# Attention and two mixing layers on one core: the first batch's Fourier transform moves into the attention loop

## The chip, the cores and the metric

One core of a Trainium2 chip runs the whole program. The metric is the device time in microseconds (us) of one execution. TensorE is PE in the profile's rows (its weight loads are PEld), VectorE is DVE, ScalarE is ACT, GpSimd is POOL, and SyncE, which here only issues DMAs, is SP. Each engine works through its own instructions strictly in order, and they meet at semaphores.

## The reference

Three layers follow one another. The first is attention over two batches of eight heads, in which a query sees only the keys that fall into the same bucket of a hash:

```python
q_bits = (np.einsum('bhsd,dk->bhsk', q, proj) > 0)          # 6 bits; the same for k
mask = q_bucket[:, :, :, None] == k_bucket[:, :, None, :]
scores = np.where(mask, scale * q @ k^T, -1e9)              # S = 768, D = 64
attn = softmax(scores);  x = attn @ v                       # x: (2, 768, 512)
X = np.real(np.fft.fft(np.fft.fft(x, axis=1), axis=2))      # second layer
u = x + X;  un = (u - mean) / sqrt(var + 1e-6)              # by row
x = u + np.maximum(un @ w_ch1, 0) @ w_ch2                   # 512 -> 2048 -> 512
theta = x @ w_theta; zr = x * cos(theta); zi = x * sin(theta)   # third layer
u = x + w_tok_r @ zr + w_tok_i @ zi;  out = u + np.maximum(u @ w_ch, 0)
```

## The kernel before

All products are made of three fp32r matmuls: each operand is split into a high part and a low part, and `product` adds high times high, high times low and low times high. So nearly every tile is evicted from PSUM twice: ACT writes the high part, then DVE subtracts it from PSUM to get the low one.

**The attention loop.** `schedule()` writes one list of slots that PE, ACT, DVE and POOL all walk. There is a slot for each of the 96 tiles (16 heads of 6 tiles of 128 queries) and six more to drain; below, (h, t) is tile t of head h, and (16, t) are the draining slots. In a slot PE computes the scores of its tile (four matmuls, lines 771 and 772), transposes the exponentials of the tile two slots earlier (`eta` and `etb`, three transposes each, line 746), does a third of the product with v (lines 786, 787), and then the small units of that slot: `bits` (the hash products, in (h, 0) and (h, 1) for the next head) and `back` (transposing the result, in (h, 3) and (h, 5) for the head before). DVE takes the row maximum straight from the score bank (`negmax`, line 993), makes the tiny `affine` out of it (line 996) and evicts the low halves `ETL`; ACT takes the exponential `E` (line 626) and evicts the high halves `ETH`. `eta`, `etb`, `bits` and `back` go round a ring of three PSUM banks (4, 5, 6).

**Between the heads.** POOL scales q (line 492), splits q and k into `TOPH` and `TOPL` two heads ahead (lines 500, 502, slot t = 2), turns the evicted products `MB` into the mask rows `MR` (line 507, slot t = 1), adds up the result and writes it into `X` (`finish`, lines 516 and 519), and splits v. SP moves the pieces with DMAs from one buffer to another: `move_away`, the load of the next q and k, `move_in`, `move_mask` (`QM<-MR`, `KM<-MR`, lines 426 and 427), the load of v. A head's scores wait for its mask rows.

**Tables and W1.** In slots t = 2 and t = 5 POOL issues one DMA out of the list `early`: twelve tables of sines and cosines, then the four DMAs of 1 MB that fill `W1H`.

**The transform.** After the loop both batches are transformed one after the other. By batch: DVE folds `X` (`fold_add`, `fold_even`, `fold_odd`), ACT and DVE split it into `EH`, `EL`, `OH`, `OL`; stage one is five groups of matmuls into `TH` and `TL` (`TG = 5`); stage two is three times a cosine and a sine product, of whose difference and sum (`DS`) DVE updates `X`. The second batch is folded while the first is in stage one.

**Into the second layer's matmuls.** SP stages W1 and W2 in chunks of 256 KB (two buffers), from which POOL makes the low halves: `split_low(n_w1)` for the sixteen chunks of W1, then `rstd` of six rows of tiles (lines 573, 575), then `load_high("w2")` (four DMAs of 1 MB, line 486) and `split_low` for W2. PE starts the second layer only with

```python
            pe.wait_ge(s_high["w1"], 16 * len(highs["w1"]))
            pe.wait_ge(s_low, n_w1)
            for n in range(2, CH):
                norm_transpose(n)
```

and the first `shrink` (the product with W2) waits for the first chunk of `W2L`.

## Time and profile before

| | |
|---|---|
| runs | 804.74 us median of 3 (799.62 to 807.62) |
| profiled execution | 805.94 us, span 803.8 us |
| PE busy | 745.3 us, 93% of the span |
| DVE, ACT, POOL busy | 445.5, 318.3, 286.9 us |
| attention loop | from the first scores at 14.11 us to 262 us |
| transform | 262 us to 330.75 us, where the first matmul with W1 starts |
| second layer | 330.75 us to about 600 us, third layer to the end |

The busy time of PE is read with care: the ends of pipelined matmuls are modelled, so that neighbours overlap in the rows. Whether PE waits is seen by the idle time in brackets behind a row, and what a matmul costs by the distance to the next one. Everything after 331 us depends only on when it starts.

### The profile page before, as it was taken

What the parts mean: (1) busy time and instruction counts of PE and PEld (TensorE: products, weight loads), DVE (VectorE), ACT (ScalarE), POOL (GpSimd) and SP (SyncE); (2) the same over time, 40 slices, a digit from 0 to 9 for tenths busy, and PEclk for the clock granted to TensorE, in tenths of its full rate; (3) what the DMA queues carried; (4) which work ended last, traced back from release to release, by engine and by line L of the source; (5) the groups of instructions that cost most, each with busy time, mean ns of one, the idle gap of its engine ahead of it and who ended that gap; (6) DMA issues with size and microseconds to landing.
All of it is one profiled execution on the core that took longest, in us unless ns stands there. A gap on an engine that the chain in (4) does not pass through costs nothing.

```text
span 803.8 us, 10972 instructions
## 1 busy us (share of the span) xinstructions
PE 745.3 (93%) x3826; PEld 625.6 (78%) x3826; DVE 445.5 (55%) x770; ACT 318.3 (40%) x659; POOL 286.9 (36%) x275
## 2 busy tenths in 40 slices
PE   4999989989999769799999999999995998999998
PEld 2788888878898557688888888888874787888876
DVE  2998997889998688522212122211127565855433
ACT  2889887879899211211111111011014342322201
POOL 3788977668772376335000000200002114312100
PEclk9999999999999869799999999999998999999999
DMA  5366548733430134712000001300002231000002
GB/s 146 94 154 170 136 93 203 192 89 87 113 73 5 53 114 135 210 40 78 1 1 1 0 1 47 99 0 1 1 31 81 60 92 40 1 14 21 19 27 78
DMA packets 44679, 56.25 MB, mean 70 GB/s; under 512 B 15956, under 2 KB 27860, under 8 KB 44116
## 3 DMA queue, kind: packets, MB, share of 16 engines
q1 hardware_dynamic: 38100, 41.65, 19.3%
q0 software_dynamic: 6528, 13.92, 6.1%
q8 instruction: 32, 0.52, 0.3%
q14 instruction: 19, 0.16, 0.1%
HBM read 38.65 MB, written 3.15 MB: 52 GB/s over the span
## 4 chain that ended last, share of the span: by engine, by line
PE 75%; DVE 14%; issue 4%; DMA 3%; ACT 2%; POOL 1%; SPq 1%; ACTq 0%; POOLq 0%
PE PS L724 20%; PE PS L726 19%; PE PS L725 19%; DVE negmax L993 4%; PE PS L746 3%; DVE ETL L1003 3%; PE PS L786 3%; PE PS L771 2%; PE PS L772 2%; PE PS L787 2%; DVE affine L996 2%; DMA KM<-MR 2%; PE PS L907 1%; PE PS L914 1%; PE PS L757 1%
## 5 line engine op out<-in xcount | busy, mean ns | idle before, releaser
L1113 DVE SCALAR_TENSOR_TENSOR HL<-PS,HH 128x512 fp32r<-128x512 f32 x48 | 33.2, 692 | 188.6 <-ACT HH L687 188.6
L687 ACT ACTIVATE HH<-PS 128x512 fp32r<-128x512 f32 x48 | 28.7, 598 | 210.4 <-PE PS L726 210.4
L626 ACT ACTIVATE E<-PS,affine 128x768 f32<-128x768 f32 x96 | 95.3, 992 | 35.7 <-DVE affine L996 33.0
L993 DVE TENSOR_REDUCE negmax<-PS 128x1 f32<-128x768 f32 x96 | 90.9, 947 | 28.4 <-PE PS L772 27.5
L1003 DVE TENSOR_TENSOR ETL<-PS,ETH 128x384 fp32r<-128x384 f32 x192 | 97.1, 545 | 1.2 <-ACT ETH L619 1.2
L619 ACT ACTIVATE ETH<-PS 128x384 fp32r<-128x384 f32 x192 | 83.4, 488 | 9.6 <-PE PS L746 9.0
L746 PE MATMUL PS<-ident,E 128*128 128x128 f32 x576 | 82.1, 276 | 4.2 <-DVE ETL L1003 4.2
L771 PE MATMUL PS<-TOPH,TOPL 128*128 128x512 f32 x192 | 69.8, 364 | 9.4 <-DMA KM<-MR 9.1
L724 PE MATMUL PS<-UTH,W1H 128*128 128x512 f32 x192 | 76.8, 400 | 1.7 <-DVE UTL L1096 1.7
L786 PE MATMUL PS<-ETH,VHL 128*128 128x384 f32 x192 | 73.2, 381 | 4.9 <-ACT OS L635 4.0
L725 PE MATMUL PS<-UTL,W1H 128*128 128x512 f32 x192 | 75.9, 396 | 0.0
L726 PE MATMUL PS<-UTH,W1L 128*128 128x512 f32 x192 | 75.8, 395 | 0.0
L726 PE MATMUL PS<-W2H,HL 128*128 128x512 f32 x192 | 74.7, 389 | 0.0
L724 PE MATMUL PS<-W2H,HH 128*128 128x512 f32 x192 | 74.7, 389 | 0.0
L725 PE MATMUL PS<-W2L,HH 128*128 128x512 f32 x192 | 74.7, 389 | 0.0
L746 PEld LDWEIGHTS PS<-ident,E 128*128 128x128 f32 x576 | 65.9, 141 | 7.6 <-DVE ETL L1003 7.1
L587 POOL TENSOR_TENSOR ZF<-X,SC 128x512 f32<-128x512 f32 x24 | 30.5, 1291 | 107.2 <-ACT SC L708 107.2
L787 PE MATMUL PS<-ETL,VHL 128*128 128x384 f32 x192 | 65.2, 340 | 0.0
L772 PE MATMUL PS<-KM,QM 76*128 76x512 f32 x192 | 63.3, 349 | 0.0
L724 PE MATMUL PS<-ZH,WTH 128*128 128x512 f32 x144 | 59.9, 416 | 0.0
L507 POOL TENSOR_SCALAR MR<-MB,gamma 24x768 fp32r<-24x768 f32 x15 | 44.0, 2933 | 43.6 <-ACT MB L643 43.6
L726 PE MATMUL PS<-ZH,WTL 128*128 128x512 f32 x144 | 57.0, 396 | 0.0
(167 smaller groups left out, 1530.2 us busy)
## 6 DMA issues: line engine op xcount, KB each, us to landing
stage<-in_moe_w_ch_dram SPq DMA_DIRECT2D x36, 256.0 KB, 2.6
QK<-in_qk_dram SPq DMA_DIRECT2D x16, 384.0 KB, 4.0
W1H<-in_moe_w_ch_dram POOLq DMA_DIRECT2D x4, 1024.0 KB, 10.4
W2H<-in_moe_w_ch_dram POOLq DMA_DIRECT2D x4, 1024.0 KB, 8.8
QM<-TOPH SPq DMA_DIRECT2D x16, 192.0 KB, 3.0
KM<-TOPL SPq DMA_DIRECT2D x16, 192.0 KB, 3.6
VR<-in_v_dram SPq DMA_DIRECT2D x16, 192.0 KB, 2.8
TOPL<-QM SPq DMA_DIRECT2D x16, 192.0 KB, 2.7
```

The lines of the kernel that those rows point to most:

```text
L619: nc.scalar.activation(ETH[:, t // HALF, k * HALF:(k + 1) * HALF, (t % HALF) * P:(t % HALF + 1) * P], bank, ACT.Copy).then_inc(s_eth, 1)
L626: nc.scalar.activation(E[:, tile % NE, :], s_bank(tile)[:, 0:S], ACT.Exp, bias=affine[:, t, 1:2], scale=affine[:, t, 0:1], accum_out=esum[ ...
L724: nc.tensor.matmul(dst, hl, hr, start=start, stop=False)
L725: nc.tensor.matmul(dst, hl, lr, start=False, stop=False)
L726: return nc.tensor.matmul(dst, ll, hr, start=False, stop=stop)
L746: last = nc.tensor.transpose(bank[:, j * P:(j + 1) * P], E[:, tile % NE, (first + j) * P:(first + j + 1) * P], ident[:])
L771: nc.tensor.matmul(dst, TOPL[:, h % 3, c], TOPH[:, h % 3, lo:hi], start=True, stop=False)
L772: last = nc.tensor.matmul(dst, QM[:, h % 2, c], KM[:, h % 2, lo:hi], start=False, stop=True)
L786: nc.tensor.matmul(OT, VHL[:, h % 2, j, :], ETH[:, c, j, :], start=(j == 0), stop=False)
L787: last = nc.tensor.matmul(OT, VHL[:, h % 2, j, :], ETL[:, c, j, :], start=False, stop=(j == QT - 1))
L993: nc.vector.tensor_reduce(negmax[:, t, 1:2], s_bank(tile)[:, 0:S], AX_X, ALU.max, negate=True).then_inc(s_max, 1)
L1003: nc.vector.tensor_tensor(ETL[where], blocks(ring(unit_no[kind, h, t])[:, 0:HC]), ETH[where].bitcast(F32), ALU.subtract).then_inc(emptied[ ...
```

## The change

Batch 0 of the transform leaves the stretch behind the loop and becomes units of the loop while batch 1's heads are computed. Its fold additions are DVE work of (9, 1), (9, 2) and (9, 4); the rest of the fold and the low halves are POOL work in (9, 5), (10, 0) and (10, 2); its stage one is `s1` units in (10, 4), (11, 1), (11, 2), (11, 4), (12, 1), its stage two an `edge` unit in (12, 4) and `sin` and `cos` units in heads 13 and 14. POOL updates `X` in (13, 3), (14, 2), (15, 0). The work buffers of batch 0 lie in the place of `W1H`, so the four DMAs of `W1H` are issued in (15, 1). The ring of three banks becomes fixed banks: `eta` 4, `etb` 5, every other unit 6. The two `bits` units of a head become one that puts both halves into one bank of 56 partitions, evicted once. SP loads q and k of head h + 2 after the mask rows of head h, where it loaded those of h + 1 before them; the mask rows take four DMAs of half the length. Behind the loop POOL makes the six `rstd` before it splits W1, and loads W2H after it, as before.

```diff
 def schedule():
-    slots = [(None, None, None, [("bits", 0, i) for i in range(2)])]
+    transform = {(10, 4): ("s1", 0, 0), (11, 1): ("s1", 0, 1), (11, 2): ("s1", 0, 2), (11, 4): ("s1", 0, 3), (12, 1): ("s1", 0, 4),
+                 (12, 4): ("edge", 0, 0)}
+    for i, place in enumerate(((13, 1), (13, 2), (13, 4), (14, 1), (14, 2), (14, 4))):
+        transform[place] = ("cos" if i % 2 else "sin", 0, i // 2)
+    slots = [(None, None, None, [("bits", 0, 0)])]
...
-        if h + 1 < NH and t < 2:
-            units.append(("bits", h + 1, t))
+        if h + 1 < NH and t == 0:
+            units.append(("bits", h + 1, 0))
...
+        if (h, t) in transform:
+            units.append(transform[h, t])
...
-        def ring(u):
-
-            return PS[:, 4 + u % RING, :]
-
-
+        bank_of = {"eta": 4, "etb": 5}
         OT = PS[:, 7, 0:HC]
+
+        def bank(kind):
+            return PS[:, bank_of.get(kind, 6), :]
...
             def move_in(h):
-                sp.wait_ge(s_ring, done["bits", h, 1])
+                sp.wait_ge(s_ring, done["bits", h, 0])
...
                 move_away(h)
-                if h + 1 < NH:
-                    load_qk(h + 1)
                 move_in(h)
                 move_mask(h)
+                if h + 2 < NH:
+                    load_qk(h + 2)
...
             def mask_rows(h):
-                pool.wait_ge(emptied["bits"], 2 * (h + 1))
-                pool.wait_ge(s_mask, 32 * h)
+                pool.wait_ge(emptied["bits"], h + 1)
+                pool.wait_ge(s_mask, 64 * h)
...
+            def fold_even(b):
+                pool.wait_ge(s_fold, 2 * HALF * (b + 1))
+                nc.gpsimd.tensor_tensor(FE[b][:, :, 1:LH], AE[b][:, :, 1:LH], AE[b][:, :, DM - 1:LH:-1], ALU.add).then_inc(s_even, 1)
+                nc.gpsimd.tensor_copy(FE[b][:, :, 0:LH + 1:LH], AE[b][:, :, 0:LH + 1:LH]).then_inc(s_even, 1)
...
+            def fold_low(b):
+                pool.wait_ge(s_eh, 3 * b + 2)
+                nc.gpsimd.tensor_tensor(EL[b][:, :, 0:LH + 1], FE[b][:, :, 0:LH + 1], EH[b][:, :, 0:LH + 1].bitcast(F32),
+                                        ALU.subtract).then_inc(s_el, 1)
...
+            def update(b, t):
...
+                pool.wait_ge(s_ds, 2 * n + 2)
+                nc.gpsimd.tensor_tensor(lower, lower, DS[b][:, n % 2, :, 0:LH + 1], ALU.add).then_inc(s_u, 1)
+                nc.gpsimd.tensor_tensor(upper, upper, DS[b][:, n % 2, ::-1, 1:LH], ALU.add).then_inc(s_u, 1)
...
-            early = [(dst, src, s_table) for dst, src in tables] + [(dst, src, s_high["w1"]) for dst, src in highs["w1"]]
+            early = [(dst, src, s_table) for dst, src in tables]
...
+                if (h, t) == (9, 5):
+                    fold_even(0)
+                if (h, t) == (10, 0):
+                    fold_odd(0)
+                if (h, t) == (10, 2):
+                    fold_low(0)
+                if (h, t) in ((13, 3), (14, 2), (15, 0)):
+                    update(0, ((13, 3), (14, 2), (15, 0)).index((h, t)))
+                if (h, t) == (15, 1):
+                    pool.wait_ge(s_ring, done["cos", 0, HALF - 1])
+                    pool.wait_ge(s_u, 2 * HALF)
+                    load_high("w1")
             finish(NH - 1, 1)
+            for n in range(QT):
+                row_scale(n)
             pool.wait_ge(s_pv, 2 * NH)
             split_low(n_w1)
...
+            pool.wait_ge(s_t, TG)
+            load_high("w2")
+            pool.wait_ge(s_m, 4)
+            pool.wait_ge(s_fix, 2 * B)
+            split_low(n_w2, FT // 2)
...
-            def take_bank(u):
-
-                if u >= RING:
-                    old = units[u - RING]
-                    pe.wait_ge(emptied[old[0]], nth[old])
...
+                if previous[name] is not None:
+                    pe.wait_ge(*freed(previous[name]))
...
+                    r = h % 3
+                    product(on[0:MP, 0:HC], projH[:, 0:MP], TOPH[:, r, 0:HC], projL[:, 0:MP], TOPL[:, r, 0:HC], True, False)
+                    last = product(on[0:MP, 0:HC], projH[:, 32:PROJ], TOPH[:, r, HC:S], projL[:, 32:PROJ], TOPL[:, r, HC:S], False, True)
...
+                elif kind == "s1":
+                    m = WIDTHS[i]
+                    pe.wait_ge(s_table, 16 * len(tables))
+                    pe.wait_ge(s_eh, 3)
+                    pe.wait_ge(s_el, 3)
+                    last = (even_group if i < HALF else odd_group)(on[0:m, 0:KC], 0, i)
...
+                place = divmod(slot - 1, QT)
+                if place in ((9, 1), (9, 2), (9, 4)):
+                    fold_add(0, ((9, 1), (9, 2), (9, 4)).index(place))
+                if place == (9, 4):
+                    fold_edge(0)
...
+                if place == (15, 1):
+                    dve.wait_ge(s_ns, 1)
+                    fix_edge(0, FX)
+                if (15, 2) <= place < (16, 2):
+                    row_moments(slot - 1 - 15 * QT - 2)
```

On POOL, between two splits of v, at the turn from head 9 to head 10. Before:

```order
L537 TENSOR_TENSOR VHL<-VR,VHL 128x6x64
L516 TENSOR_TENSOR OS_68<-OL_67 128x192
L519 TENSOR_TENSOR X<-OS_68,einv 128x3x64
L507 TENSOR_SCALAR MR<-MB,gamma 24x768
L492 TENSOR_SCALAR QK<-QK 64x768
L500 CAST TOPH<-QK 128x768
L502 TENSOR_TENSOR TOPL<-QK,TOPH 128x768
```

And in the changed kernel, behind the same split of v:

```order
L547 TENSOR_TENSOR FE_114<-AE_112 128x3x255
L548 COPY FE_114<-AE_112 128x3x2
L583 TENSOR_TENSOR OS_68<-OL_67 128x192
L586 TENSOR_TENSOR X<-OS_68,einv 128x3x64
L551 TENSOR_TENSOR FO_115<-AO_113 128x3x255
L543 TENSOR_SCALAR MR<-MB,gamma 56x384
L528 TENSOR_SCALAR QK<-QK 64x768
L536 CAST TOPH<-QK 128x768
L538 TENSOR_TENSOR TOPL<-QK,TOPH 128x768
L555 TENSOR_TENSOR EL_117<-FE_114,EH_116 128x3x257
L557 TENSOR_TENSOR XL<-FX,XH 1x257
L559 TENSOR_TENSOR OL_119<-FO_115,OH_118 128x3x255
```

Two operations of the fold stand around `finish`, and the three low halves behind the split of q and k.

On PE, slot (10, 4) of the changed kernel, from its transposes on, followed by the scores of (10, 5):

```order
L847 MATMUL PS<-ident,E 128x128 x6
L902 MATMUL PS<-ETH,VHL 128x384
L903 MATMUL PS<-ETL,VHL 128x384
...
L811 MATMUL PS<-ALT,XH 128x386
L812 MATMUL PS<-ALT,XL 128x386
L805 MATMUL PS<-CSH,EH_116 128x386
L806 MATMUL PS<-CSL,EH_116 128x386
L807 MATMUL PS<-CSH,EL_117 128x386
...
L887 MATMUL PS<-TOPH,TOPL 128x512
```

The first group of stage one now stands in PE's row ahead of the next tile's scores; before, the scores follow directly upon line 787.

On POOL, from the last `finish` to W2. Before:

```order
L519 TENSOR_TENSOR X<-OS_68,einv 128x3x64
L528 TENSOR_TENSOR W1L<-stage,W1H 128x512 x16
L573 TENSOR_SCALAR rstd<-moments 128x1
L575 TENSOR_TENSOR rstd<-rstd,mhalf 128x1
...
L486 DMA W2H<-in_moe_w_ch_dram 128x4x512 x4
L528 TENSOR_TENSOR W2L<-stage,W2H 128x512 x8
```

In the changed kernel:

```order
L586 TENSOR_TENSOR X<-OS_68,einv 128x3x64
L572 TENSOR_SCALAR rstd<-moments 128x1
L574 TENSOR_TENSOR rstd<-rstd,mhalf 128x1
...
L595 TENSOR_TENSOR W1L<-stage,W1H 128x512 x16
L522 DMA W2H<-in_moe_w_ch_dram 128x4x512 x4
L595 TENSOR_TENSOR W2L<-stage,W2H 128x512 x8
```

The six pairs of `rstd` have moved from behind the sixteen splits to the front of them.

## Rows read from the trace of the kernel before

**Rows 1.** Windows: start:end, length, busy us (instructions) by engine, granted clock, DMA share, GB/s.
```profile
220.00:240.00 20.00, 19.77 (x134) 18.08 (x133) 18.57 (x35) 18.27 (x43) 13.88 (x11) 1.00 0.31 76
262.00:331.00 69.00, 50.44 (x239) 39.09 (x239) 54.09 (x86) 14.94 (x31) 36.98 (x37) 0.80 0.41 130
```

**Rows 2.** Timeline of PE: scores of (12, 5) and of (13, 0).
```profile
213.34 0.40 PE L771 MATMUL PS<-TOPH,TOPL 128*128 128x512 f32 x1
...
216.12 0.48 PE L771 MATMUL PS<-TOPH,TOPL 128*128 128x512 f32 x1
```

**Rows 3.** Timeline of POOL: the mask rows made in heads 6, 10 and 11.
```profile
111.15 2.93 POOL L507 TENSOR_SCALAR MR<-MB,gamma 24x768 fp32r<-24x768 f32 x1 [4.32 <-ACT MB L643]
...
179.00 2.93 POOL L507 TENSOR_SCALAR MR<-MB,gamma 24x768 fp32r<-24x768 f32 x1 [5.20 <-ACT MB L643]
...
193.61 2.93 POOL L507 TENSOR_SCALAR MR<-MB,gamma 24x768 fp32r<-24x768 f32 x1 [2.91 <-ACT MB L643]
```

**Rows 4.** Timeline of POOL and the chain of waits, heads 7 to 9.
```profile
118.97 0.62 POOL L561 DMA_DIRECT2D W1H<-in_moe_w_ch_dram  x1
...
150.64 2.13 POOL L492 TENSOR_SCALAR QK<-QK 64x768 f32<-64x768 f32 x1 [3.78 <-DMA QK<-in_qk_dram]
...
130.74 4.54 DMA KM<-MR
```

**Rows 5.** Timelines of POOL and DVE: the split of k beside `affine`.
```profile
99.94 1.82 POOL L502 TENSOR_TENSOR TOPL<-QK,TOPH 128x768 fp32r<-128x768 f32 x1
...
100.08 1.69 DVE L996 SCALAR_TENSOR_TENSOR affine<-negmax 128x2 f32<-128x2 f32 x1
...
215.29 0.80 DVE L996 SCALAR_TENSOR_TENSOR affine<-negmax 128x2 f32<-128x2 f32 x1
```

**Rows 6.** Timeline of SP: issue of the first mask rows.
```profile
10.84 0.83 SPq L426 DMA_DIRECT2D QM<-MR  x1
```

**Rows 7.** Timeline of PE: batch 1's stage one and stage two, first and last matmul.
```profile
303.82 0.44 PE L815 MATMUL PS<-ALT,XH 1*128 1x386 f32 x1
...
313.52 0.34 PE L726 MATMUL PS<-SSH,OL 128*127 128x386 f32 x1
...
316.15 0.37 PE L724 MATMUL PS<-CDH,TH 128*128 128x258 f32 x1
...
323.54 0.28 PE L726 MATMUL PS<-SDH,TL 127*128 127x258 f32 x1
```

**Rows 8.** Timeline of DVE: batch 0's fold, first and last but one.
```profile
262.66 1.75 DVE L952 TENSOR_TENSOR AE<-X 128x1536 f32<-128x1536 f32 x1
...
269.54 0.41 DVE L972 TENSOR_TENSOR XL<-FX,XH 1x257 fp32r<-1x257 f32 x1
```

**Rows 9.** Groups of instructions, whole span: POOL's high parts, DVE's `row_moments`.
```profile
L500 POOL CAST TOPH<-QK 128x768 fp32r<-128x768 f32 x15 | 12.3, 823 | 1.0
...
L1030 DVE BATCH_NORM_STATS2 stats<-X 128x6 f32<-128x512 f32 x12 | 8.1, 677 | 0.0
```

**Rows 10.** Timeline of PE: a start after a wait, and the last product with v.
```profile
135.52 0.76 PE L771 MATMUL PS<-TOPH,TOPL 128*128 128x512 f32 x1 [1.59 <-DMA KM<-MR]
...
265.33 0.34 PE L787 MATMUL PS<-ETL,VHL 128*128 128x384 f32 x1
```

**Rows 11.** Timeline of POOL behind the loop.
```profile
276.25 2.53 POOL L528 TENSOR_TENSOR W1L<-stage,W1H 128x512 fp32r<-128x512 f32 x2 [2.75 <-DMA stage<-in_moe_w_ch_dram]
...
309.94 0.23 POOL L573 TENSOR_SCALAR rstd<-moments 128x1 f32<-128x1 f32 x1
...
315.68 3.10 POOL L486 DMA_DIRECT2D W2H<-in_moe_w_ch_dram  x4
329.89 2.68 POOL L528 TENSOR_TENSOR W2L<-stage,W2H 128x512 fp32r<-128x512 f32 x2 [11.11 <-issue]
```

**Rows 12.** Timeline of PE: the first matmuls with W1 and with W2.
```profile
330.75 0.76 PE L724 MATMUL PS<-UTH,W1H 128*128 128x512 f32 x1 [1.70 <-DVE UTL L1096]
...
339.19 0.39 PE L724 MATMUL PS<-W2H,HH 128*128 128x512 f32 x1
```

More of the change, by code:

```diff
@@ L128, in program @@
     TOPL = put("TOPL", [P, 3, S], F32R)
+    MX = put("MX", [1, 2, DM])
+    assert used[0] <= dft_at + 4 * 4 * QT * KC
     used[0] = dft_at + 4 * 4 * QT * KC
@@ L220, in program @@
             units += us
-        unit_no = {u: i for i, u in enumerate(units)}
-        done = {}
+        done, previous, last_on = {}, {}, {}
         for u in units:
             done[u] = len(done) + 1
+            k = bank_of.get(u[0], 6)
+            previous[u] = last_on.get(k)
+            last_on[k] = u
         nth, seen = {}, {}
@@ L251, in program, with freed @@
         s_x = sem("s_x")
+        def freed(u):
+            if u[0] in emptied:
+                return emptied[u[0]], nth[u]
+            return {"s1": (s_tl, nth[u]), "sin": (s_bs, nth[u]), "cos": (s_ds, 2 * nth[u]), "edge": (s_ns, 1)}[u[0]]
         s_mr = sem("s_mr")
@@ L439, in _ @@
             load_v(1)
+            load_qk(2)
             n = 0
@@ L642, in _ @@
                             act.wait_ge(s_mr, h - 1)
[L643 removed]
+                        nc.scalar.activation(MB[:], bank(kind)[0:MP, 0:HC], ACT.Copy).then_inc(emptied["bits"], 1)
                     elif kind == "back":
@@ new lines, in _ @@
+                if slot - 1 == 10 * QT + 1:
+                    high_even(0)
+                if slot - 1 == 10 * QT + 2:
+                    high_odd(0)
+            high_even(1)
+            high_odd(1)
+            for g in range(TG):
+                m = WIDTHS[g]
+                act.wait_ge(s_t, g + 1)
+                nc.scalar.activation(TH[1][0:m, g, :], PS[0:m, g % 2, 0:KC], ACT.Copy).then_inc(s_th, 1)
+            for t in range(HALF):
+                n = HALF + t
+                act.wait_ge(s_m, t + 1 + (t > 0))
+                act.wait_ge(s_ds, 2 * (n - 1))
+                nc.scalar.activation(BS[1][:, n % 2, 0:LH + 1], PS[:, 4 + n % 2, 0:LH + 1], ACT.Copy).then_inc(s_bs, 1)
@@ new lines, in _ @@
+            for g in range(TG):
+                m = WIDTHS[g]
+                pe.wait_ge(s_eh, 3 + (2 if g < HALF else 3))
+                pe.wait_ge(s_el, 3 + (2 if g < HALF else 3))
+                if g >= 2:
+                    pe.wait_ge(s_tl, TG + g - 1)
+                (even_group if g < HALF else odd_group)(PS[0:m, g % 2, 0:KC], 1, g).then_inc(s_t, 1)
+            pe.wait_ge(s_th, TG * B)
+            pe.wait_ge(s_tl, TG * B)
+            pe.wait_ge(emptied["back"], seen["back"])
+            pe.wait_ge(emptied["pv"], 2 * NH)
@@ new lines, in _ @@
+            for g in range(TG):
+                m = WIDTHS[g]
+                dve.wait_ge(s_th, TG + g + 1)
+                nc.vector.tensor_tensor(TL[1][0:m, g, :], PS[0:m, g % 2, 0:KC], TH[1][0:m, g, :].bitcast(F32), ALU.subtract).then_inc(s_tl, 1)
+                if g < 2:
+                    normalize(g)
+            normalize(2)
+            normalize(3)
+            for t in range(HALF):
+                n = HALF + t
+                two = X[:, QT + t:2 * QT:HALF, :]
+                lower, upper = two[:, :, 0:LH + 1], two[:, :, DM - 1:LH:-1]
+                differences(1, t, PS[:, 2 + n % 2, :])
+                dve.wait_ge(s_ds, 2 * n + 2)
+                nc.vector.tensor_tensor(lower, lower, DS[1][:, n % 2, :, 0:LH + 1], ALU.add).then_inc(s_u, 1)
+                nc.vector.tensor_tensor(upper, upper, DS[1][:, n % 2, ::-1, 1:LH], ALU.add).then_inc(s_u, 1)
+                if t == 0:
+                    dve.wait_ge(s_m, 2)
+                    fix_edge(1, PS[0:1, 1, :])
```

410 lines of the change are left out of this document (193 added, 217 removed).

## The prediction

> **What bounds the kernel now.** I read the windows first. In a head of the loop that nothing disturbs, PE is busy 19.77 of 20 us, DVE 18.57, ACT 18.27 and POOL 13.88, at the full clock of 2.4 GHz [rows 1]: the loop is bound by PE, and DVE stands close behind (about 1.0 us free in a head). Then the timeline of POOL's mask rows, as a metronome: one head lasts 14.61 us (179.00 to 193.61), but the four before it took 67.85 us (111.15 to 179.00) where 58.44 were due: 9.4 us of waiting [rows 3]. The chain of waits and POOL's timeline name the cause: the first DMA of W1H is issued at 118.97, then mask rows take 4.54 us to land and a load of q and k holds POOL for 3.78 us [rows 4]. Last, the stretch behind the loop, 262 to 331 us: PE is busy 50.44 of 69 us at a mean granted clock of 0.80, POOL 36.98 [rows 1]. The reader is to see there which engine would be last if the first batch's transform were gone: not PE, as worked out below.
>
> **Part 1, what enters the loop.** PE: stage one of a batch took 303.82 to 313.7, 9.9 us, and stage two 316.15 to 323.7, 7.5 us, both at the full clock [rows 7]. PE has next to no idle time in the loop, so these 17.4 us are paid in full. The evictions of these units on ACT and DVE (stage one 0.5 us each, estimated from the widths) stand in slots that the units themselves lengthen by 1 to 2.3 us; I put them at 0. POOL's six updates of X, some 1.2 us each by TOPL's 1.82 us for 768 columns [rows 5], lie in POOL's free time: 0 as well, between 0 and 4 us.
>
> Head 9: DVE gets the additions, 2 times 1.75 us in all [rows 8], and some 0.8 us for the edge row: 4.3 us in a head with 1.0 us free, so 3.3 us on the path. Bounds 1 (the tiles in flight absorb part) and 6 (each addition also waits for POOL, next part but one).
>
> Slot (10, 4): PE's first stage-one group waits for `OL`, the last of a row of POOL work that starts when DVE has done its additions of (9, 4), about when head 10 begins. In POOL's order: FE 1.9, `finish` 1.1, FO 1.8, MR 1.5 (half of 2.93, as half the columns), QK 2.13, TOPH 0.82, TOPL 1.82, EL 1.85, XL 0.6, OL 1.8; the fold's operations priced by TOPL's rate, `finish` as two of 192 columns [rows 3, 4, 5, 9]. That is 15.3 us. PE reaches its place after 11.8 us: head 12 began at 216.12 less 14.61 = 201.51, and its sixth tile's scores stand at 213.34 [rows 2]. PE waits 3.5 us, and everybody behind it: the scores of (10, 5) are queued after that group. Bounds 1 and 7. After a wait of 1.59 us the first matmul took 0.76 us instead of 0.40 [rows 2, 10], the low clock of 1.2 GHz; I add 1.7 us for that, between 0 and 5.
>
> Head 15: `row_moments` of four tiles at 0.68 us [rows 9] and the repair of the edge row give DVE 3.5 us, while PE there has no hash products: 1.5 us, between 0 and 3.5.
>
> The start: before the first scores the mask rows need two more DMA issues at 0.83 us [rows 6]: 1.6 us. Later heads don't pay it, as the rows come earlier: one `bits` unit instead of two, and 1.5 us of MR instead of 2.93 [rows 3]. The single eviction of MB saves ACT, which is not the bound: 0.
>
> **Part 2, what leaves the loop.** The four DMAs of W1H, and with them the 9.4 us of waiting [rows 3, 4]. The loads of q and k move behind the mask rows of SP's row, so the mask rows pass one transfer of 384 KB earlier and q and k arrive a head before their use. The tables stay where they are. At 100.08 an `affine` of two columns took 1.69 us, until POOL's split at 99.94 had ended [rows 5]; that split now falls elsewhere in the head, and I count half of those 1.5 us as gone. Together 10.2 us saved; bounds 7 and 12.5.
>
> Loop: 17.4 + 3.3 + 3.5 + 1.7 + 1.5 + 1.6 - 10.2 = +18.8 us.
>
> **Part 3, behind the loop** (in the old trace's times, as if the loop ended at the same time). The last product with v ends at 265.7 [rows 10]. ACT is no longer blocked by the first batch's fold, so two evictions, a transpose and `finish` complete X at about 268.5 (2.8 us, an estimate). Then two rows run side by side.
>
> PE's: the fold of batch 1, which batch 0's stage one no longer hides, 262.66 to 269.95 before, 7.3 us [rows 8], gives 275.8; from the first stage-one matmul to the first with W1 it was 303.82 to 330.75, 26.9 us [rows 7, 12]; with 2 us for a low clock at the start, 304.7.
>
> POOL's: six `rstd`, 309.94 to 315.68, 5.7 us, to 274.2; sixteen splits of W1, 276.25 to 309.94, 33.7 us, to 307.9 [rows 11]. This is later than PE's row, and PE may transpose its last two tiles only behind it: some 3.6 us more, 311.5, and the two first `hidden` groups take 330.75 to 339.19, 8.4 us [rows 12]: ready for W2 at 319.9. But POOL issues W2H only behind those splits: it took 315.68 to 329.89, 14.2 us, to land, and the first split 1.3 us [rows 11]. So the first matmul with W2 stands at 323.4 instead of 339.19 [rows 12]: 15.8 us saved, less 1.7 us for a low clock after a 3.5 us wait: -14.1 us. Of the 28 us and more that a batch's transform costs behind the loop, the other half goes to POOL's row, which is as long as before and only starts earlier.
>
> **Sum.** 18.8 - 14.1 = +4.7 us. The profiled execution took 805.94 us (span 803.8 and 2.1 around it) and would take 810.6. It lies 1.2 us above the median, so the prediction for the median is 804.74 + 4.7 = 809.4 us.
>
> **A rule that speaks against the change.** What the row shows: an `affine`, which reads two small tiles in SBUF, took 1.69 us beside POOL's TOPL and ended with it, and 0.80 us in the undisturbed head [rows 5]. The change puts eleven more such operations on POOL, and six additions with two SBUF inputs on DVE, into the loop; I priced what they may hold up by the bounds of head 9 and by rival A. The Trainium skill ("SBUF — State Buffer", section "Who interferes with whom") says that a VectorE instruction with two SBUF inputs and a GpSimd instruction that reads SBUF exclude each other, the later one blocking until the other has ended; the row at 100.08 agrees. If it holds for every one of the eleven, the result is rival A's.
>
> **The rivals.**
> A, slower: `affine` is held up more often. `eta` and `etb` used to have a third bank to run into; now the transposes of a tile wait for DVE's eviction of the tile before, so that a delay on DVE reaches PE one unit sooner. For it: DVE is free only 1.0 us in a head, TOPL lasts 1.82 us of a slot that has 14.61 / 6 = 2.4, and it meets other tiles than before, since MR starts a slot earlier and is 1.5 us shorter [rows 1, 3, 5]. Against it: POOL has 1.5 us less in each head. From about 0.6 us a head it decides; at that, 14 heads lose 8.4 us: 818 us.
> B, faster by the loop: fold and low halves fit in, 1 us in head 9 and 1 us at (10, 4) with no low clock, none in head 15, and 12.5 us of waits go. Loop +8.5, behind it -15.8 as PE keeps its clock: 797.5 us.
> C, POOL's row is not last: without competition for SBUF from DVE the sixteen splits go at 1.26 us each and the loads keep up, ending by 300. Then PE's row decides, W1 at 304.7, W2H lands by 314.5: first W2 matmul at 316, 7 us earlier: 802 us. Against it: the splits wait for the staging DMAs (2.75 us before the first [rows 11]), not for POOL alone.
> D, the units don't run beside anything: nothing else is gained at all, W1's waits return with the table DMAs. That is +9.4 on the forecast, 819 us; little speaks for it.
>
> **How the numbers follow.** Forecast 0.47, A 0.22, B 0.17, C 0.10, D 0.04. The forecast's own range is 803 to 815. A measurement of this kernel tells a change of about 1%, 8 us, from none: under 796.7 is faster, over 812.8 slower. B falls half on either side of 796.7 and widens it downwards: faster 0.13. A and D and the upper end of the forecast are slower: 0.33. Same 0.54. The range takes in most of A and B: 797 to 819.
>
> **What would show it.** The mask rows' metronome is even from head 2 on, without the gaps of 111 to 179 us. In slot (10, 4) PE waits for POOL's `OL` by 3 to 4 us, and not before. Head 9 lasts about 18 us. Between the loop and W1's first matmul PE waits for POOL's last split of W1, with an idle time of 5 us or more, and the first matmul with W2 waits for `W2L`. The first matmul with W1 stands 49 to 50 us behind DVE's last eviction of the loop (68 before). I would be wrong if the heads' period moves by more than 0.5 us, or if the splits of W1 end before PE's row does.

## The result, and the profile after

The changed kernel takes 827.92 us (median of 4 runs, 824.28 to 829.34), the kernel before 805.59 us (median of 4) beside it. The ratio is 1.028, 95% interval 1.022 to 1.035: 2.8% slower, outside the range of the prediction. The profiled execution took 829.34 us, its span is 826.8 us against 803.8 and its mean granted clock 0.963 against 0.968.

Four marks cut both traces at the same places: the mask rows (`MR` on POOL) as the metronome of the heads, the last product with v, the first matmul with W2, the end. Times in us:

| stretch | before | after | difference | forecast |
|---|---|---|---|---|
| start to the mask rows of (1, 1) | 35.02 | 38.57 | +3.55 | +1.6 |
| heads 1 to 8 | 125.24 | 124.26 | -0.98 | -6.1 |
| heads 9 to 13 | 77.17 | 98.87 | +21.70 | with the next row |
| (14, 1) to the last product with v | 27.90 | 36.88 | +8.98 | +23.3, both rows |
| to the first matmul with W2 | 73.86 | 61.56 | -12.30 | -15.8 |
| to the end | 464.6 | 466.7 | +2.1 | +1.7 |

(The forecast of -10.2 for the waits is divided by where the waits lay: 5.3 us of the 9.4 in heads 6 to 8 and the `affine` in head 5, the other 4.1 in head 9.) The loop lost 33.25 us where 18.8 were forecast; the stretches behind it gained 10.2 where 14.1 were forecast. Most of the 2.1 us at the end is the low clock behind PE's wait for W2: 0.60 from 360 to 364 us, where it was 1.00 before. Heads 1 to 8 show the loss best, since they have nothing of the transform in them. Timeline of POOL in the changed kernel, the mask rows made in slots (4, 1), (5, 1), (9, 1) and (10, 1):

```profile
85.20 1.65 POOL L543 TENSOR_SCALAR MR<-MB,gamma 56x384 fp32r<-56x384 f32 x1 [1.79 <-ACT MB L712]
100.73 1.65 POOL L543 TENSOR_SCALAR MR<-MB,gamma 56x384 fp32r<-56x384 f32 x1 [1.78 <-ACT MB L712]
...
162.83 1.66 POOL L543 TENSOR_SCALAR MR<-MB,gamma 56x384 fp32r<-56x384 f32 x1 [1.79 <-ACT MB L712]
186.15 1.66 POOL L543 TENSOR_SCALAR MR<-MB,gamma 56x384 fp32r<-56x384 f32 x1 [1.37 <-ACT MB L712]
```

A head lasts 15.53 us (85.20 to 100.73), and heads 1 to 8 all lie between 15.50 and 15.56; before it was 14.61 [rows 3]. So the gaps are gone, as forecast, and 0.92 us more in every head have taken their place. (One more gap is gone, of 2.6 us in head 5, which the prediction did not count: before, the mask rows of (5, 1) and (6, 1) stand at 93.91 and 111.15, ahead of the first DMA of W1H.) Head 9, with the fold additions, lasts 23.32 us.

Inside such a head, timeline of PE: the first matmul of the scores of (4, 1), behind the bits unit, to that of (5, 1), and one wait between them:

```profile
84.41 0.39 PE L887 MATMUL PS<-TOPH,TOPL 128*128 128x512 f32 x1
...
86.47 0.39 PE L887 MATMUL PS<-TOPH,TOPL 128*128 128x512 f32 x1
...
88.87 0.39 PE L887 MATMUL PS<-TOPH,TOPL 128*128 128x512 f32 x1
...
91.17 0.48 PE L887 MATMUL PS<-TOPH,TOPL 128*128 128x512 f32 x1
...
92.34 1.01 PE L847 MATMUL PS<-ident,E 128*128 128x128 f32 x6 [0.23 <-DVE ETL L1101]
...
93.90 0.39 PE L887 MATMUL PS<-TOPH,TOPL 128*128 128x512 f32 x1
...
96.74 0.48 PE L887 MATMUL PS<-TOPH,TOPL 128*128 128x512 f32 x1
...
99.93 0.39 PE L887 MATMUL PS<-TOPH,TOPL 128*128 128x512 f32 x1
```

The reader is to see the distances: 2.06, 2.40, 2.30, 2.73, 2.84, 3.19 us. A slot in which PE waits for nothing and that holds no unit is 2.06; a `back` adds 0.24, the six matmuls of the bits 1.04. Six slots, two `back` and the bits make 13.88 us, so PE stands still for 1.65 us of the head, against 0.73 before by the same count. DVE in the same head:

```profile
85.31 0.96 DVE L1091 TENSOR_REDUCE negmax<-PS 128x1 f32<-128x768 f32 x1 [0.95 <-PE PS L888]
...
89.77 0.96 DVE L1091 TENSOR_REDUCE negmax<-PS 128x1 f32<-128x768 f32 x1 [0.31 <-PE PS L888]
90.76 1.05 DVE L1094 SCALAR_TENSOR_TENSOR affine<-negmax 128x2 f32<-128x2 f32 x1
...
97.73 0.96 DVE L1091 TENSOR_REDUCE negmax<-PS 128x1 f32<-128x768 f32 x1 [0.67 <-PE PS L888]
```

DVE waits 0.95 us for scores, with all six bits matmuls in front of them on PE, and again 0.31 and 0.67; then PE waits for DVE. Neither has more work than before; they take turns in waiting. The table of waits, whole span, what waited, for whom, us, times, longest:

```profile
ACT E L698 <- DVE affine L1094: 43.3, 31, 14.8
DVE negmax L1091 <- PE PS L888: 40.0, 39, 8.3
...
PE PS L847 <- DVE ETL L1101: 12.6, 21, 3.3
...
PE PS L887 <- DMA KM<-MR: 7.3, 1, 7.3
```

PE's transposes wait for `ETL` 12.6 us in 21 places. For the mask rows PE waits once, before the first scores, and no longer in the middle as in [rows 10].

Head 9, timelines of DVE, POOL and PE:

```profile
175.34 1.51 DVE L1041 TENSOR_TENSOR AO<-X 128x512 f32<-128x512 f32 x1
176.77 0.40 DVE L1049 TENSOR_TENSOR FX<-X 1x255 f32<-1x255 f32 x1
177.11 1.76 DVE L1050 COPY FX<-X 1x2 f32<-1x2 f32 x1
...
176.93 1.92 POOL L547 TENSOR_TENSOR FE<-AE 128x765 f32<-128x765 f32 x1 [0.63 <-DVE AO L1041]
...
180.78 1.54 PE L847 MATMUL PS<-ident,E 128*128 128x128 f32 x6 [3.27 <-DVE ETL L1101]
```

A copy of two numbers on one partition took 1.76 us, until POOL's fold had ended, where the same copy takes 0.15 us behind the loop. After the wait of 3.27 us PE's matmuls run at the low clock of 1.2 GHz until 186.6 us (0.52 us for a bits matmul instead of 0.34).

Behind the loop, timelines of PE and POOL (with the last product with v, PE's wait for the last split of W1, the last `finish` and the third `rstd`):

```profile
298.58 0.33 PE L903 MATMUL PS<-ETL,VHL 128*128 128x384 f32 x1
...
309.94 0.66 PE L811 MATMUL PS<-ALT,XH 1*128 1x386 f32 x1 [9.83 <-DVE XL L1157]
...
344.72 1.94 PE L914 MATMUL PS<-ident,UN 128*128 128x128 f32 x8 [10.78 <-POOL W1L L595]
...
348.41 0.76 PE L805 MATMUL PS<-UTH,W1H 128*128 128x512 f32 x1 [1.74 <-DVE UTL L1185]
...
360.14 0.47 PE L805 MATMUL PS<-W2H,HH 128*128 128x512 f32 x1 [3.40 <-POOL W2L L595]
```

```profile
301.38 0.51 POOL L586 TENSOR_TENSOR X<-OS,einv 128x192 f32<-128x192 f32 x1
301.98 0.72 POOL L572 TENSOR_SCALAR rstd<-moments 128x1 f32<-128x1 f32 x1
...
305.53 2.70 POOL L572 TENSOR_SCALAR rstd<-moments 128x1 f32<-128x1 f32 x1
...
312.94 2.49 POOL L595 TENSOR_TENSOR W1L<-stage,W1H 128x512 fp32r<-128x512 f32 x2
...
344.30 3.12 POOL L522 DMA_DIRECT2D W2H<-in_moe_w_ch_dram  x4
358.74 2.50 POOL L595 TENSOR_TENSOR W2L<-stage,W2H 128x512 fp32r<-128x512 f32 x2 [11.33 <-DMA W2H<-in_moe_w_ch_dram]
```

These answer to [rows 7, 11, 12]. POOL's row is the last, step for step as forecast: PE waits 10.78 us for the last split of W1 and 3.40 us for `W2L`. Only the `rstd` took 11.0 us (301.98 to 312.94), not 5.7: the first four pairs, each one column wide, stand beside DVE's fold.

### The profile page after: what moved, and what is told of

It is laid out like the page before. It is cut to its first block, busy times and chain, and to the rows that moved or that the text cites. A ratio compares the mean times of both kernels' runs of the same rounds, so it can differ in the third digit from the quotient of the medians.

```text
span 826.8 us, 10977 instructions
## 1 busy us (share of the span) xinstructions
PE 752.6 (91%) x3826; PEld 628.8 (76%) x3826; DVE 431.7 (52%) x765; ACT 317.5 (38%) x645; POOL 284.2 (34%) x287
## 4 chain that ended last, share of the span: by engine, by line
PE 60%; POOL 20%; issue 11%; DMA 5%; DVE 2%; SPq 1%; ACT 1%; POOLq 0%
PE PS L805 18%; PE PS L807 17%; PE PS L806 17%; POOL QK L528 3%; DMA stage<-in_moe_w_ch_dram 3%; POOL TOPL L538 2%; POOL MR L543 2%; POOL OS L583 2%; PE PS L847 2%; POOL W1L L595 1%; DMA W2H<-in_moe_w_ch_dram 1%; POOL VHL L604 1%; POOL TOPH L536 1%; PE PS L998 1%; POOL X L586 1%
## 5 line engine op out<-in xcount | busy, mean ns | idle before, releaser
L847 PE MATMUL PS<-ident,E 128*128 128x128 f32 x576 | 87.3, 284 | 12.7 <-DVE ETL L1101 12.6
L847 PEld LDWEIGHTS PS<-ident,E 128*128 128x128 f32 x576 | 65.4, 144 | 23.3 <-DVE ETL L1101 22.3
L806 PE MATMUL PS<-ZL,WTH 128*128 128x512 f32 x144 | 56.8, 395 | 0.0
```

Of the source, the lines that this page charges most:

```text
L806: nc.tensor.matmul(dst, hl, lr, start=False, stop=False)
L847: last = nc.tensor.transpose(on[:, j * P:(j + 1) * P], E[:, tile % NE, (first + j) * P:(first + j + 1) * P], ident[:])
```

## The experiments

In the diffs lines of either kernel are cut to what changes. The head period is always the distance of the mask rows; "heads" are those without transform work.

### Which part makes the head longer

**Fixed banks alone, in the kernel before.**

```diff
-            return PS[:, 4 + u % RING, :]
+            return PS[:, bank_of.get(units[u][0], 6), :]
...
-                if u >= RING:
-                    old = units[u - RING]
+                old = previous[units[u]]
+                if old is not None:
```

> The kernel before with one part of the change alone: eta always in bank 4, etb in bank 5, bits and back in bank 6, in place of the ring of three. Theory 1 (the fixed banks cost the 0.92 us by which every undisturbed head grew, 15.53 against 14.61 us between two mask rows): the heads of this kernel grow by 0.6 to 1.0 us and the time by 10 to 15 us, to 816 to 821 us. Theory 2 (the heads grew because POOL's split of q and k now meets other affines, through the one bits unit and the shorter mask rows): nothing of that is in this kernel, the heads stay at 14.6 us and the time at 804 to 808 us.

808.96 us, ratio 1.005 (1.001 to 1.010). The period is 15.31 us, +0.70, in most heads and 15.4 to 15.6 in the others, as theory 1 had it, but the time is not: it gave 816 to 821 us. The gaps of 111 to 179 us vanish in the longer heads, so that the whole costs only 4 us; in the profiled execution, the fastest of this kernel, the last product with v even stands at 264.44, 0.9 us earlier than in [rows 10]. Fixed banks alone make a head longer, and a longer head hides late mask rows.

**The ring of three back, in the changed kernel** (`4 + k`, `k = len(done) % 3`, for all units; the bits stay one unit).

> The changed kernel with the ring of three banks given back to all units, the transform's too. Theory 1: heads 2 to 8 fall from 15.53 to 14.6 us, and the later ones by as much or more; 828 us become 811 to 816 us. Theory 2: 826 to 829 us, heads unchanged.

825.08 us, ratio 1.027 (1.019 to 1.036); heads 15.54 us as before the edit. So the banks are not all that holds the changed kernel's heads: something else gives the same period by itself.

**Both bits units in one slot, in the kernel before.**

```diff
-        if h + 1 < NH and t < 2:
-            units.append(("bits", h + 1, t))
+        if h + 1 < NH and t == 0:
+            units += [("bits", h + 1, 0), ("bits", h + 1, 1)]
```

> The kernel before, with one edit: both bits units of a head stand in slot t = 0 on PE, where the second stood in t = 1. Ring of three, two evictions, 24 mask rows and everything else stay. Theory 2a (the slots of PE are now uneven: a slot with six more matmuls of 384 columns lets ACT and DVE run dry and the next ones are short): heads go from 14.61 us towards 15.5 us, the time to 812 to 818 us. Theory 2b (not the place on PE but the merged bank, its 56 partitions and POOL's row behind it cost the 0.9 us a head): heads stay at 14.6 us, the time within 3 us of before.

819.87 us, ratio 1.025 (1.020 to 1.030); heads 16.0 to 16.3 us, more than either theory gave. The same matmuls and evictions, one slot earlier, cost 1.4 to 1.7 us a head. (Two units in one slot also go round the ring in another order, so part of it may be the ring's.)

**Ring of three and two bits units, in the changed kernel** (schedule, tiles of 24 rows, two evictions and two mask DMAs as in the kernel before).

> The changed kernel with the ring of three banks and with the two bits units of before (t = 0 and t = 1, 24 mask rows, two evictions, two mask DMAs); transform of the first batch in the loop, q and k two heads ahead, late W1H as in the changed kernel. Theory 2 (merging the bits, by place or by phase, costs the 0.9 us a head once the banks are a ring again): heads at 14.61 us, time 825 less 14 times 0.93, about 812 us. Rival (something else of the change, for instance q and k two heads ahead, moves POOL's row): heads stay at 15.5 us, time 825 us.

822.31 us, ratio 1.028 (1.022 to 1.033). Heads 14.6 to 14.9 us: with both undone the period is the old one, so that q and k loaded two heads ahead and late W1H have no part in its growth. (The four mask DMAs and the mask rows of 56 partitions were undone with the merged unit and were not tried alone.) But the ratio did not move, for heads 9 and 10 grew to 23.7 and 25.6. Timeline of PE in slot (10, 4) of this kernel:

```profile
188.59 0.65 PE L809 MATMUL PS<-ALT,XH 1*128 1x386 f32 x1 [6.05 <-POOL OL L557]
```

This is the wait that the prediction priced at 3.5 us, and the low clock behind it (0.65 us). In the changed kernel the same matmul waits 0.36 us: its own heads are late enough to hide it.

**POOL's split one slot later** (`scale_q` and `split_top` behind `finish` in t = 3; ring of three, one bits unit).

> The changed kernel with the ring of three banks and one unit of bits, and with POOL's scaling of q and its split of q and k one slot later (t = 3, behind finish). Theory 2b (phase: POOL's TOPL of 1.82 us meets an affine and holds it up at the point where PE has least in hand): heads change by 0.3 us or more in either direction, most likely back towards 14.6, time 812 to 820 us. Theory 2a (PE's uneven slots): heads stay at 15.5 us within 0.1, time 823 to 827 us.

823.67 us, ratio 1.029 (1.024 to 1.034); heads 15.53 to 15.77 but for one of 17.0 and one of 14.9. Which `affine` POOL's split holds up is not what sets the period; whether it would be shorter if none were held up was not tried.

**Two bits units, fixed banks kept, in the changed kernel.**

> The changed kernel with the fixed banks kept and only the bits unit undone: two units in t = 0 and t = 1 as before, both in bank 6. Theory (fixed banks are enough for a longer head: with two banks for eta and etb each transpose waits for DVE's eviction of the tile before): heads 15.3 us as with fixed banks in the kernel before, time 823 to 828 us. Rival (in the changed kernel the bits unit alone sets the head): heads at 14.6 to 14.9 us, time 814 to 820 us.

836.43 us, ratio 1.040 (1.033 to 1.046), slower than the changed kernel. Heads 15.3 to 15.5 us, as the theory had it for them; but PE waits 6.06 us for `OL` in (10, 4), and in five places, 5.4 us in all and 1.21 us at most, for the eviction of `MB`, since a bits unit now follows another unit in bank 6, and heads 9 to 13 take 110.3 us instead of 98.9. I had not thought of that bank.

Together: fixed banks give 15.3, the single bits unit 15.5, both 15.53, neither 14.61. Each is enough and they don't add.

### Heads 9 and 10

**Stage one a little later, in the changed kernel** (first group in (11, 1) instead of (10, 4), the others behind it).

> The changed kernel with the five stage-one units moved to (11,1), (11,2), (11,4), (12,1), (12,2), so that the first of them no longer follows POOL's low halves by less than a slot. If PE's place at (10,4) cost what was forecast (3.5 us and a low clock), 3 to 5 us are gained: 823 to 825 us. If the cost of heads 9 and 10 lies in DVE's additions and in what POOL holds up, POOL's low halves ending early enough for a PE that is late anyway, the time stays within 2 us of 828 us.

827.26 us, ratio 1.030 (1.023 to 1.037), and 99.0 us for heads 9 to 13 instead of 98.9: nothing. The forecast wait of 3.5 us in (10, 4), with its 1.7 us of low clock, is not where this kernel loses.

**The fold additions one to a slot, in the changed kernel.**

```diff
-                if place in ((9, 1), (9, 2), (9, 4)):
-                    fold_add(0, ((9, 1), (9, 2), (9, 4)).index(place))
-                if place == (9, 4):
+                if (9, 1) <= place < (10, 1):
+                    fold_add(0, *divmod(slot - 1 - 9 * QT - 1, 2))
+                if place == (10, 1):
                     fold_edge(0)
```

with POOL's fold in (10, 1), (10, 3), (10, 5) and stage one from (11, 1).

> The changed kernel (fixed banks, one bits unit, rstd behind the loop) with the six fold additions one to a slot in (9, 1) to (10, 0), the edge row in (10, 1), POOL's fold in (10, 1), (10, 3), (10, 5) and stage one from (11, 1). Theory P (head 9 is long because two additions in a row, and three ops on the edge row, stand between an affine and the next eviction, and PE has no bank to run into): heads 9 and 10 together take 35 to 38 us instead of 43.2, time 820 to 824 us. Rival (DVE's work is what it is, 4.3 us or more with the blocking, in a head that is full): heads 9 and 10 together 41 to 43 us, time as the changed kernel, 825 to 828 us.

823.69 us, ratio 1.028 (1.021 to 1.034). Heads 9 and 10 take 18.46 and 20.16, 38.6 us together instead of 43.2: between the two expectations. The two numbers are not quite alike, for this edit also moves a stage-one group out of (10, 4). Over heads 9 to 13, out of which nothing moves, it is 94.1 us instead of 98.9, and instead of 99.0 in the kernel with stage one later and nothing else: in the traces 4.8 us came from bunching. The measured times cannot confirm it, since the intervals of the two ratios overlap almost wholly.

### The DMAs

**W1H late, in the kernel before** (its four DMAs issued in (15, 1)).

> The kernel before with one part of the change alone: the four DMAs of W1H are issued in slot (15,1) instead of slots 2 and 5 of heads 7 and 8. If those DMAs caused the 9.4 us of waiting between 111 and 179 us of the trace before, the time falls by 7 to 10 us to 796 to 799 us and the mask rows come every 14.6 us from there on. Rival: the waiting stems from the loads of q and k, issued right ahead of the mask rows, and W1H only adds to it: less than 4 us are gained.

800.35 us, ratio 0.996 (0.991 to 1.000), above the 796 to 799 expected. The gaps of W1H are gone, one of 4.1 us stays between the mask rows of (5, 1) and (6, 1), where 2.6 us stood before. The last product with v stands 7.0 us earlier than in [rows 10] (258.31), the first matmul with W2 6.2 us earlier than in [rows 12] (333.00).

**W1H late and q and k two heads ahead, in the kernel before** (with a load for head 2 ahead of the loop).

```diff
                 move_away(h)
-                if h + 1 < NH:
-                    load_qk(h + 1)
                 move_in(h)
                 move_mask(h)
+                if h + 2 < NH:
+                    load_qk(h + 2)
```

> The kernel before with W1H loaded in (15, 1) and with q and k loaded two heads ahead behind the mask rows, nothing else. Theory (the gap of 4.1 us that late W1H alone left in head 6 is q and k coming late behind the table DMAs; loaded a head earlier they are there): all heads within 0.4 us of 14.6, the last mask rows at about 226 us, the time 4 us below late W1H alone: 794 to 799 us, ratio 0.988 to 0.994. Rival (the DMAs of the tables hold up whatever load or mask row stands beside them): a gap of 3 us or more stays in heads 4 to 7, ratio 0.994 to 0.999.

796.74 us (796.51 without one execution of 4127 us), ratio 0.994 (0.990 to 0.998, without that one), the lowest ratio here, though its interval overlaps almost wholly with that of W1H late alone. All heads from 2 on are 14.6 to 14.9 us, the last mask rows stand at 225.64 instead of 237.43: 11.8 us saved in the loop, where the forecast had 10.2. In the profiled execution (803.31 us, at the upper end of this kernel's) 5.0 us are left at the first matmul with W2 (334.23 against 339.19), where W1H late alone had left 6.2. What differs in between is the clock: 0.70 on average in the 69 us from 250.2, where [rows 1] have 0.80 for as long a stretch. The longest waits of PE there are nearly the same as before, among them 4.87 us for ACT's `OS` (4.88 before). What held the clock down was not tested.

### Behind the loop

**`rstd` in the loop, in the changed kernel** (`row_scale` in (15, 3) to (16, 2)).

> The changed kernel with one edit: POOL makes the six rstd of the first batch inside the loop, in (15, 3) to (16, 2), and not behind it. Theory T (POOL's row behind the loop sets the first matmul with W2, and the rstd stand 11 us in it, held up beside the fold of the second batch): the W1 splits start and end 8 to 11 us earlier, the time is 817 to 820 us. Rival (the splits are held by something else, their staging DMAs or by DVE's use of SBUF during the fold, so what rstd gives up the splits lose): 823 to 828 us.

818.84 us, ratio 1.023 (1.017 to 1.029). Timeline of POOL, the first splits:

```profile
298.75 3.12 POOL L595 TENSOR_TENSOR W1L<-stage,W1H 128x512 fp32r<-128x512 f32 x2 [2.80 <-DMA stage<-in_moe_w_ch_dram]
303.21 4.21 POOL L595 TENSOR_TENSOR W1L<-stage,W1H 128x512 fp32r<-128x512 f32 x2 [1.34 <-DMA stage<-in_moe_w_ch_dram]
```

The splits start 2.8 us behind the last `finish` instead of 11.0, but now it is they that stand beside the fold: two of them take 4.21 us instead of 2.5, and DVE's fold makes PE wait 13.68 us, not 9.83. From the last `finish` to the first matmul with W2 it is 52.7 us instead of 58.3: of 8.2 us given up 5.6 arrive. PE no longer waits for the last split of W1, and only 0.88 us for `W2L`: POOL's row and PE's now end almost together. The time fell by 9 us, into the range expected, but the kernel before was faster in this comparison too (801.41 us): the ratio fell from 1.028 to 1.023, about 4 us, and the two intervals overlap.

**W2H after the tenth split, besides.**

```diff
-            split_low(n_w1)
+            split_low(n_w1, 10)
             pool.wait_ge(s_t, TG)
             load_high("w2")
+            split_low(n_w1)
```

> The changed kernel with the six rstd in the loop (as in the experiment on rstd) and, besides, the four DMAs of W2H issued after the tenth of the sixteen W1 splits instead of after the last. Theory T (POOL's row sets the first matmul with W2 and W2H's 14 us stand in it alone): the DMAs land during the last splits, PE's wait for W2L before the first matmul with W2 is gone, and the time falls by 3 to 8 us below the experiment on rstd (818.8 us), so 811 to 816 us. Rival (DMA transfers share bandwidth: the 4 MB slow the staging of the last six W1 chunks by as much as they save): W1 is split 4 us or more later and the time stays at 817 to 820 us.

821.51 us, ratio 1.025 (1.020 to 1.031). Timelines of POOL and PE:

```profile
324.27 3.27 POOL L522 DMA_DIRECT2D W2H<-in_moe_w_ch_dram  x4 [2.98 <-PE PS L808]
327.55 2.74 POOL L595 TENSOR_TENSOR W1L<-stage,W1H 128x512 fp32r<-128x512 f32 x2
335.00 1.26 POOL L595 TENSOR_TENSOR W1L<-stage,W1H 128x512 fp32r<-128x512 f32 x1 [4.71 <-DMA stage<-in_moe_w_ch_dram]
...
343.56 1.94 PE L915 MATMUL PS<-ident,UN 128*128 128x128 f32 x8 [9.88 <-POOL W1L L595]
```

The time is that of the rival or a little more: the sixteen splits and what stands between them take 42.8 us instead of 33.4. Its reason covers a part only. Of the 9.4 us POOL spends 2.98 waiting for PE's stage one, which the line ahead of `load_high` asks for, and 3.27 issuing the four DMAs; the rest is staging beside the 4 MB, where one DMA of 256 KB took 6.2 us to land (median 2.6) and kept POOL waiting 4.71 us. PE waits 9.88 us for W1 where it had waited 0.88 us for W2.

### All repairs

**Ring, two bits units, fold spread, `rstd` in the loop, W2H after ten splits.**

> The changed kernel with every repair that the runs so far point to: ring of three banks, two bits units in t = 0 and t = 1, the six fold additions of the first batch one to a slot in (9, 1) to (10, 0) with the edge row in (10, 1) and everything behind it a head later (stage one from (11, 2)), rstd in the loop, W2H issued after ten W1 splits. Theory (PE's units of 17.4 us are paid in full in the loop, and nothing else need be lost): heads at 14.61 us, head 9 at 17 us, heads 10 to 14 together 73 + 17 = 90 us against 95 to 104 before, time 797 to 803 us, the same as the kernel before within 1%. Rival (DVE and POOL exclude each other on SBUF for every fold operation wherever it stands): heads 9 and 10 still lose 8 us together, time 806 to 812 us.

808.04 us, ratio 1.009 (1.006 to 1.012), in the rival's range. Heads are 14.6 us, but heads 9 and 10 take 18.34 and 19.62, together 8.8 us above two undisturbed ones, though no unit of the transform stands in them on PE. Here the mask rows mislead as a metronome. POOL is busy 19.2 of the 19.6 us of head 10, and makes the rows of (11, 1) 1.5 us after their `MB` is there (190.89 against 189.35). By PE's own scores of (9, 1), (10, 1) and (11, 1), at 148.91, 166.55 and 184.44, the two heads take 17.64 and 17.89, 6.3 us above two undisturbed ones. Windows of these two heads (busy us of PE, PEld, DVE, ACT, POOL, then clock, DMA share and GB/s), and of head 9 in the kernel before with the two DMA edits:

```profile
148.91:166.55 17.64, 15.31 (x97) 13.08 (x97) 17.40 (x31) 13.20 (x30) 12.68 (x12) 1.00 0.34 84
166.55:184.44 17.89, 15.56 (x97) 13.07 (x97) 15.79 (x31) 13.68 (x31) 13.06 (x11) 1.00 0.32 82
...
148.60:163.20 14.60, 14.38 (x97) 13.11 (x97) 13.75 (x27) 13.21 (x30) 11.28 (x11) 1.00 0.40 101
```

DVE is busy 17.40 of head 9's 17.64 us, and 5.7 us longer in the two heads than in two undisturbed ones. The fold's own operations on it are 5.1 us of that. So the rival's mechanism, DVE and POOL shutting each other out, is there (single `affine` take 1.3 us beside POOL's `MR` and 1.0 beside its `FE`, 0.16 alone), but it is the smaller part.

**The same with W2H behind all splits.**

> As the kernel with every repair, but W2H is loaded behind all sixteen W1 splits, as in the changed kernel; so it is the kernel before with the first batch's transform in the loop, spread as evenly as it was found to go, with late W1H, q and k two heads ahead and rstd in the loop. Theory (W2H in the middle cost more than it gave: with it the sixteen splits and their gaps took 42 us, without it 33 us; the first matmul with W2 stood 52.9 us behind the first split against 49.9 us): 3 us less than the kernel with every repair, 804 to 806 us beside a before of 804, ratio 1.001 to 1.008; the transform in the loop gives back what it takes and wins nothing. Rival (PE's row sets the first matmul with W2, whatever POOL does): within 1 us of the kernel with every repair.

806.29 us, ratio 1.004 (1.002 to 1.007), the ratio within what was expected. This is the kernel before with the transform of batch 0 in the loop at the least loss found. In its trace the last product with v stands at 283.48, 18.2 us later than before [rows 10], and the first matmul with W2 at 338.38, 0.8 us earlier than [rows 12]: 54.9 us behind the loop instead of 73.9. Against the kernel before, moving the transform gives back what it takes. But this kernel also has the two DMA edits, and these alone gave a ratio of 0.994: beside its proper partner the transform in the loop loses about 1% (1.004 against 0.994, the intervals apart). In the two traces the last product with v stands 29.9 us later (283.48 against 253.57) and the first matmul with W2 4.2 us later (338.38 against 334.23).

The 29.9 us, by PE's scores: 0.9 to (1, 1), 0.0 in heads 1 to 8, 6.4 in heads 9 and 10 (the fold), 16.2 in heads 11 to 13 (stage one, the edge and half of stage two), 6.4 from (14, 1) on.

## Why the prediction was wrong

**The step that failed** is in part 1: the head was taken to stay at 14.61 us. "The single eviction of MB saves ACT, which is not the bound: 0" priced the merged bits unit by the engines' busy sums, and the fixed banks were left to a rival. Measured, each makes an undisturbed head 0.7 to 0.9 us longer. Over 15 heads 0.92 us are 13.8 us, about the 14.4 by which the loop exceeded its forecast; the other misses, below, nearly cancel. The prediction's own sign of being wrong (that the heads' period moves by more than 0.5 us) is what happened. Undoing it by itself brought no time back, though (ratio 1.028 in both): with heads of 14.6 us the wait in (10, 4) came in, at 6.05 us, and heads 9 and 10 grew by 6.1 us together.

**What was right** shows in the last kernel above, in which the period is the old one and the fold is spread: its last product with v stands 18.2 us later than before (forecast 18.8), its span is 1.6 us longer (forecast 4.7). The forecast described that kernel; part of the agreement is luck, as its terms show below.

**Rival A** named the right place, a lost third bank, and its right consequence. It was given 0.6 us a head, 818 us and a chance of 0.22. The fixed banks were measured at 0.70. What it missed is the bits unit: with the ring of three back the period stayed at 15.54, and POOL's split moved by a slot left it there. That the merged unit does it is shown by undoing it (with its mask rows and four DMAs), and that its place is enough by the two units in one slot of the kernel before, but for the order of the ring. How the uneven slot costs time (DVE starves behind the long slot and is late for the short ones) is read from the rows of one head and is argued, not shown.

**The rule on SBUF** (Trainium skill, "SBUF — State Buffer", "Who interferes with whom"): the trace agrees for the `rstd` at 305.53, which took 2.70 us beside DVE operations with two SBUF inputs and ended when the last of these had (308.23 and 308.14). The copy of two numbers at 177.11 reads one tile; for such operations the section has another case, that a copy can take the shared ports too, and the row agrees with it in so far as the copy ended when POOL's `FE` did (178.87 and 178.85). I had weighed the rule for `affine` only. It cost most where rows of tiny operations of one engine stood beside big ones of the other: at the end of head 9 and in the `rstd`.

**Head 9** was priced at 3.3 us, bounds 1 to 6; it is 7.8 (23.32 less 15.53), beyond the bound, with the low clock in it. Nor does it end there: head 10 is longer too. In the repaired kernel the fold costs 6.3 us in both heads together, by PE's scores. It was priced as DVE's 4.3 us less 1.0 us that DVE had free. Measured, its operations on DVE are 5.1 us, what POOL holds up adds to them, and none of the free time was used. ACT's three high parts of the fold (`EH`, `XH`, `OH`, 2.1 us) stand in no term of the prediction; what they cost was not tested. And the prediction never set POOL's 15.3 us row against a head that keeps POOL busy for 10 of 14.61 us already.

**Slot (10, 4)**: forecast 3.5 us and 1.7 for the clock; 0.36 in the changed kernel, 6.05 where the heads are short. The chain on POOL was right, but it was priced against PE in heads of 14.61 us; in the changed kernel PE itself comes late to its place, and the wait is hidden.

**Head 15 and the units**: (14, 1) to the last product grew by 8.98 us, and by 6.4 where the period is the old one. Half of stage two is 3 to 4 us of that, so about 3 us are left for head 15 (forecast 1.5, bounds 0 to 3.5); whether DVE's `row_moments` are the reason was not taken apart. The units themselves were paid in full, as forecast, and a little more: 16.2 us in heads 11 to 13 for what the rates of [rows 7] put at about 14.

**The start** was forecast at +1.6 us. PE's first scores stand at 16.49 instead of 14.11, +2.4. To the mask rows of (1, 1) it was +3.55 in this execution, and between -1.4 and +1.5 in four other kernels with the same start; what makes head 0 last 12.9 to 17.6 us is open.

**W1H's gaps**: forecast 10.2 us saved. In size that is right, as the experiment without the transform shows (11.8), but W1H is not the whole cause: late W1H alone gave 7.0 us at the last mask rows, and q and k two heads ahead the other 4.8, among them the gap ahead of W1H's first DMA. And in the changed kernel the slower heads would have swallowed the gaps anyway, as they did with fixed banks alone. The forecast booked a gain of 10.2 that a slower loop had already taken.

**Behind the loop**: -15.8 forecast and -12.3 measured, and +2.1 at the low clock behind it (forecast 1.7); POOL's row last, as forecast, so rival C is out. `rstd` 11.0 us instead of 5.7, the sixteen splits 31.4 instead of 33.7, from the last split to W2 with its first split 15.8 (forecast 15.5).

## What to carry to other kernels

In a loop where PE, DVE and ACT hand one tile round and each is over 90% busy, the period is set by who waits for whom inside a slot, not by the sums: price a merged unit or a bank less by the distances of the slots, and try it alone first. A loop that gets slower hides late transfers and late rows of another engine, so once the period grows, removing them gains nothing more. A row of one engine that serves as a metronome is late itself where that engine is full: check it against the engine that does the work. Compare a change with the kernel that has its side edits alone, not only with the old one: here the side edits hid a loss of 1%. Work taken out of a stretch shortens it only down to the next engine's row, and taking the head off that row can set it against work it did not meet before.

## What I had not expected of the hardware

POOL's `MR` took 1.65 us for 56 x 384 and 2.93 for 24 x 768 [rows 3]: its time went with the columns, not with the partitions. An operation of one or two columns takes 0.15 to 0.22 us alone and 1.76 us (DVE's copy, beside POOL's `FE`) or 2.70 us (POOL's `rstd`, beside a row of six operations of DVE's fold). Beside four DMAs of 1 MB a staging DMA of 256 KB took 6.2 us to land, where the median is 2.6.
